# Ten of sixteen FFN weight slabs are loaded and split in the first FFN block instead of six of them in attention and four there

## What is computed

```python
# 1. attention: 4 batches, 8 heads, 576 positions, head size 64
out_d = sm_attn(q_d, k_d, v_d)              # on means of 4 positions
out_up = np.repeat(out_d, 4, axis=2)
mask = np.abs(pos[:, None] - pos[None, :]) < 4
out_local = np.matmul(softmax(where(mask, scale * q @ k.T, -1e9)), v)
x = out_up + out_local                      # 2304 tokens x 512
# 2. FFN: w_in 512 x 2048, w_out 2048 x 512
h = x @ w_in
g = h * np.tanh(log1p(exp(h)))
x = g @ w_out
# 3. each token goes through the best of 8 experts (512 x 1024, 1024 x 512)
```

## Time and profile before

| | us |
|---|---|
| median of 3 runs (946.82 to 948.1) | 946.95 |
| span of the profiled execution | 947.0 |
| TensorE busy | 871.4 (92%) |
| DVE busy | 510.1 (54%) |
| ACT busy | 429.1 (45%) |
| POOL busy | 231.5 (24%) |
| attention, to the first ffn_in | 0 to 214.5 |
| first FFN block, to the first ffn_out of the second | 214.5 to 291.5 |

### The profile page before, as it was taken

One profiled execution on the slowest core, in us unless ns is written; L12 is line 12 of the kernel. 1 busy time (PEld: TensorE's weight loads), 2 busy tenths in 40 slices (PEclk: granted clock), 3 DMA queues, 4 the chain that ended last, 5 costly groups with the idle time before them and its releaser, 6 DMA issues.

```text
span 947.0 us, 16050 instructions
## 1 busy us (share of the span) xinstructions
PE 871.4 (92%) x4845; PEld 734.7 (78%) x4846; DVE 510.1 (54%) x1023; ACT 429.1 (45%) x1186; POOL 231.5 (24%) x218
## 2 busy tenths in 40 slices
PE   4888888879999999999999999987799999999995
PEld 3666666668988988989989989975577777777773
DVE  6999999945756555555555555675741111111110
ACT  3777777754555445454454454452152222222121
POOL 2667666542230010010010001252311111111110
PEclk9899999969999999999999999998899999999997
DMA  5555555211100000000000000310331011110110
GB/s 117 149 147 149 148 148 147 56 43 45 45 1 34 1 1 33 0 0 33 0 0 33 0 0 34 115 64 34 127 107 45 22 44 44 43 39 28 44 44 12
DMA packets 88197, 51.57 MB, mean 54 GB/s; under 512 B 64480, under 2 KB 77280, under 8 KB 88160
## 3 DMA queue, kind: packets, MB, share of 16 engines
q1 hardware_dynamic: 85040, 41.16, 15.5%
q0 software_dynamic: 3120, 9.96, 3.1%
HBM read 41.67 MB, written 9.70 MB: 54 GB/s over the span
## 4 chain that ended last, share of the span: by engine, by line
PE 67%; DVE 14%; issue 6%; DMA 5%; ACT 3%; POOL 2%; DVEq 1%; SPq 0%; ACTq 0%; POOLq 0%
PE ps L1326 7%; PE ps L1327 7%; PE ps L1328 7%; PE ps L1302 6%; PE ps L1301 6%; PE ps L1307 6%; PE ps L1436 6%; PE ps L1438 6%; PE ps L1437 6%; DMA xg<-y_rows,gidx 4%; DVE smax L889 3%; DVE ssum L899 3%; DVE kdz L874 2%; DMA vwin<-in_v_dram 2%; PE ps L1227 1%
## 5 line engine op out<-in xcount | busy, mean ns | idle before, releaser
L988 DVE TENSOR_SCALAR Tb<-Eb 128x384 f32<-128x384 f32 x96 | 41.4, 431 | 133.9 <-ACT Eb L733 133.9
L733 ACT ACTIVATE Eb<-ps 128x384 f32<-128x384 f32 x96 | 47.1, 491 | 141.7 <-PE ps L1307 141.6
L1302 PE MATMUL ps<-xh,WA 128*128 128x384 f32 x288 | 98.3, 341 | 0.0
L663 ACT ACTIVATE prob<-ps,nmax 96x111 f32<-96x111 f32 (+1 forms) x256 | 87.8, 356 | 23.0 <-DVE nmax L893 22.7
L1301 PE MATMUL ps<-xh,WA 128*128 128x384 f32 x288 | 97.8, 340 | 0.0
L562 POOL TENSOR_TENSOR xl<-xT,xh 128x384 fp32r<-128x384 f32 x24 | 26.8, 1144 | 280.4 <-ACT xh L705 280.4
L1326 PE MATMUL ps<-WA,gh 128*128 128x512 f32 x216 | 87.1, 403 | 2.4 <-DVE gl L947 2.4
L1328 PE MATMUL ps<-WA,gl 128*128 128x512 f32 x216 | 85.4, 395 | 0.0
L1327 PE MATMUL ps<-WA,gh 128*128 128x512 f32 x216 | 85.2, 394 | 0.0
L1167 DVE TENSOR_TENSOR hTl<-ps,hTh 128x1024 fp32r<-128x1024 f32 x19 | 23.3, 1225 | 112.5 <-ACT hTh L796 112.5
L742 ACT ACTIVATE Rb<-Tb 128x384 f32<-128x384 f32 x96 | 50.5, 526 | 73.6 <-DVE Tb L990 73.6
(11 more groups left out here) (218 smaller groups left out, 2078.6 us busy)
## 6 DMA issues: line engine op xcount, KB each, us to landing
wsraw<-in_moe_w_dram SPq DMA_DIRECT2D x32, 256.0 KB, 3.2
vwin<-in_v_dram SPq DMA_DIRECT2D x32, 166.5 KB
qraw<-in_q_dram SPq DMA_DIRECT2D x32, 144.0 KB, 3.0
kraw<-in_k_dram SPq DMA_DIRECT2D x32, 144.0 KB, 3.1
vdraw<-in_v_dram SPq DMA_DIRECT2D x32, 144.0 KB
y_rows<-yrow SPq DMA_DIRECT2D x6, 768.0 KB, 3.6
wraw<-in_moe_w_in_dram SPq DMA_DIRECT2D x12, 256.0 KB, 5.6
wraw<-in_moe_w_out_dram SPq DMA_DIRECT2D x12, 256.0 KB, 3.5
```

Source lines behind the costliest of these rows:

```text
L663: last = act.activation(prob[0:np_, a.s6, n * w:(n + 1) * w], ps[0:np_, o:o + w], ACT.Exp, scale=sc, bias=nmax[0:np_, a.s6, n:n + 1], accu ...
L1302: pe.matmul(dst, lo, xh[:, kk, :], start=False, stop=False)
```

## The change

Only slabs 0 to 5 (NPRE = 6) are still loaded in attention, one in every second pair, into a wraw of half the size. Slabs 6 to 15 are loaded behind attention, and ACT casts one at the end of each of the first ten steps of the first FFN block. yrow and yT become one tensor, ystage, which is two stage buffers for slabs before it is used as yrow and yT; so two late slabs can be in flight. ACT gets a wait for w_lo ahead of the first xh, since xh lies where attention's buffers were. Where the parts of a slab lie (WA, WB) and what TensorE does stays.

```diff
-        wraw = alloc(att, "wraw", [P, 2, 2 * DM])
+        wraw = alloc(att, "wraw", [P, 2 * DM])
...
-        yrow = alloc(early, "yrow", [P, NS, DM])
-        yT = alloc(early, "yT", [P, NK, P])
+        ystage = alloc(early, "ystage", [P, NS * DM + NK * P])
+        yrow = ystage[:, 0:NS * DM].rearrange("p (s n) -> p s n", s=NS)
+        yT = ystage[:, NS * DM:NS * DM + NK * P].rearrange("p (a b) -> p a b", a=NK)
+        def slab_stage(j):
+            return ystage[:, (j % 2) * 2 * DM:(j % 2 + 1) * 2 * DM]
...
-        SLAB_LAG = 2
+        NPRE = NPAIR // 2 - 2
         def has_slab(m):
-            return not isinstance(m, int) or SLAB_LAG <= 2 * m < NWA + SLAB_LAG
+            return not isinstance(m, int) or 1 <= m <= NPRE
...
-                j, par = hp * B + (n - V_LAG), (n - V_LAG) % 2
-                split = hp * B + (n - V_LAG - 1)
                 load_v(hp, n - V_LAG)
-                if not static or j < NWA:
-                    wait(sp, w_lo, split)
-                    load_slab(j, wraw[:, par], wraw_in[par])
+                if (n - V_LAG) % 2 == 0:
+                    j = hp * (B // 2) + (n - V_LAG) // 2
+                    if not static or j < NPRE:
+                        wait(sp, w_lo, j)
+                        load_slab(j, wraw, wraw_in)
...
-            for j in range(NWA, NF):
-                sp.wait_ge(w_lo, j)
-                load_slab(j, yrow[:, 0:2, :].rearrange("p a b -> p (a b)"), wraw_in[j % 2])
+            for j in range(NPRE, NF):
+                wait(sp, w_lo, max(NPRE, j - 1))
+                load_slab(j, slab_stage(j), late_in[j % 2])
...
-                if has_slab(m) and dn % 3 == 1:
-                    split_lo(m * 2 + (dn // 3 - SLAB_LAG), wraw[:, dn // 3], True)
+                if has_slab(m) and dn == 1:
+                    split_lo(m - 1, wraw, True)
...
                 act.wait_ge(pooled, ROUNDS * NPAIR)
+                act.wait_ge(w_lo, NPRE)
                 x_part_hi(0)
...
-                    if first_block and j % 3 == 2 and NWA + j // 3 < NF:
-                        late_slab_hi(NWA + j // 3)
+                    if first_block and NPRE + j < NF:
+                        late_slab_hi(NPRE + j)
```

More of the change, by code:

```diff
@@ L133, in build @@
         Rb = alloc(early, "Rb", [P, 2, TB])
-        yrow = alloc(early, "yrow", [P, NS, DM])
-        yT = alloc(early, "yT", [P, NK, P])
+        ystage = alloc(early, "ystage", [P, NS * DM + NK * P])
+        yrow = ystage[:, 0:NS * DM].rearrange("p (s n) -> p s n", s=NS)
+        yT = ystage[:, NS * DM:NS * DM + NK * P].rearrange("p (a b) -> p a b", a=NK)
+        assert NS * DM + NK * P == 2 * (2 * DM)
+        def slab_stage(j):
+            return ystage[:, (j % 2) * 2 * DM:(j % 2 + 1) * 2 * DM]
         early.close()
@@ L273, in build @@
         v_due = sem("v_due")
-        wraw_in = [sem("wraw_in0"), sem("wraw_in1")]
+        wraw_in = sem("wraw_in")
+        late_in = [sem("late_in0"), sem("late_in1")]
         w_hi = sem("w_hi")
@@ L565, in _ @@
             x_part_lo(0)
-            for j in range(NWA, NF):
-                split_lo(j, yrow[:, 0:2, :].rearrange("p a b -> p (a b)"))
+            for j in range(NPRE, NF):
+                split_lo(j, slab_stage(j))
             with pool.Fori(1, NTB) as i:
@@ L746, in ffn_block @@
                         y_evac(i - 1)
-                    if first_block and j % 3 == 2 and NWA + j // 3 < NF:
-                        late_slab_hi(NWA + j // 3)
+                    if first_block and NPRE + j < NF:
+                        late_slab_hi(NPRE + j)
             def late_slab_hi(j):
-                split_hi(j, yrow[:, 0:2, :].rearrange("p a b -> p (a b)"), wraw_in[j % 2], 32 * (j // 2) + 32)
+                split_hi(j, slab_stage(j), late_in[j % 2], 32 * ((j - NPRE) // 2) + 32)
             def g_part_hi(c, par):
@@ L929, in step @@
                     copy_turned(dve.tensor_copy, dve, a, DVE_ROUND)
-                if has_slab(m) and dn % 3 == 0:
-                    j, par = m * 2 + (dn // 3 - SLAB_LAG), dn // 3
-                    dve.wait_ge(wraw_in[par], m * 32)
+                if has_slab(m) and dn == 0:
+                    dve.wait_ge(wraw_in, m * 32)
                     for which in range(2):
-                        last = dve.tensor_copy(w_part(j, which, 0, True), wraw[:, par, which * DM:(which + 1) * DM])
+                        last = dve.tensor_copy(w_part(m - 1, which, 0, True), wraw[:, which * DM:(which + 1) * DM])
                     last.then_inc(w_hi, 1)
```

## The result

The changed kernel takes 960.62 us (median of 4 runs, 957.95 to 963.65), the kernel before 946.88 (946.5 to 948.1). The ratio is 1.0149, with a 95% interval of 1.0123 to 1.0175: 13.7 us slower. The forecast was 960.3, in a range of 954 to 963. The profiled execution after spans 960.0 us against 947.0.

A forecast was written before the change was run, and what follows sets the result against it. Attention was taken as bound by the value-load loop over SP, loads and POOL, the FFN blocks by TensorE. 947.0 - 0.9 (attention) + 14.2 (first FFN block) = 960.3 us, range 954 to 963.

The forecast's parts named there:

- The sum, 960.3 us: Whole kernel: 947.0 us before, less 0.9 in attention, plus 14.2 in the first FFN block; own case 958.5 to 962.5, chance 0.70.
- Attention, -0.9 us: Attention: six slabs fewer to load and split gain 0.9 us, the middle between bounds of 0 and 1.7.
- the loop of the loads: Attention: vdraw and vwin loads issued by SP, their landing and POOL's additions form one loop of 11.92 us a pair.
- Rival 1: Attention: DVE sets the pace, so each of six pairs gains 1.2 us, 7.2 in all, giving 954.0 us; chance 0.14.
- Rival 2: Attention: SP's queue sets the pace; some 3.3 us of slab issue leaves each of six pairs, giving 941.3 us; chance 0.03.
- One sign: Attention, profile after: POOL's sums (L524's successor) were to be 11.6 to 12.0 us apart in all pairs.
- The first slab, +4.3 us: First FFN block's start: ACT waits 1.7 us for the first late slab, so ffn_out(0) starts 4.3 us late, at 227.7.
- Nine steps of 5.30 us: First FFN block, ffn_out(0) to ffn_out(9): steps of 5.30 us against TensorE's 4.19; ffn_out(9) at 275.4 instead of 261.15.
- Rival 3: First FFN block: the slab work is hidden in each step, only the start loses 2.8 us, giving 948.9 us; chance 0.04.
- The clock, 0 to 1.6 us: First FFN block: TensorE's clock may fall during its first wait, costing 1.6 us at most; 0 was taken.
- Rival 4: First FFN block: the clock stays at 1.2 GHz beyond the first gap, +4 us a step, +42 over ten; chance 0.06.

## Why the prediction was right, point by point

**The sum, 960.3 us.** It missed the median by 0.3 us. The four runs spread over 5.7 us, so a hit as close as that is luck; that the loss is 12 to 17 us is not. The prediction took span and time as one, but in the runs on record the time is 1.7 to 2.0 us above the span. It did no harm, as 947.0 was the median of the times too.

**Attention, -0.9 us.** 1.1 us measured at the first ffn_in, and 0.2 us as the mean of three kernels with the same attention. The bounds of 0 and 1.7 held it; that the middle came so near is luck. The upper bound put the 0.29 us by which the last three pairs are shorter down to the slabs. They are 11.45 us apart after the change and the twelve before them 11.88, so the lead is not smaller with half the slabs gone: it isn't theirs, and zero was the right bound. That the loop of the loads sets the pace in the kernel before and the changed one is shown from three sides: opening it in either of two places shortens a pair (to 10.06 and 10.97 us), slowing its load lengthens the pair by 6.0 us, by as much as SP's issue of the load (9.31 instead of 3.35) and by as much as the load by the estimate, and taking slabs from DVE does nothing that shows. Rival 1 falls. Rival 2, a slab's issue on SP as the price, falls with the same rows: the pairs without a slab aren't 2.4 us shorter, POOL idles longer in them. One sign was set too narrow: the sums on POOL were to be 11.6 to 12.0 us apart in all pairs. They are 11.36 to 12.83 apart, and were 11.39 to 12.42 before.

**The first slab, +4.3 us.** ACT waited 1.48 us (forecast 1.7); ffn_out(0) started 4.75 us behind the cast (4.80), at 226.90, 13.51 us after the first ffn_in, before 8.90: 4.6 us. Moving the casts one step later took 3.6 of them back.

**Nine steps of 5.30 us.** ffn_out(9) came at 274.57. The forecast had 275.4 less the 0.9 of attention, 274.5. Against the first ffn_in it is 14.5 us late, forecast 14.2; the 0.3 us are the first slab's. The reading of the last block, where the same pattern stood already, gave this number to 0.1 us a step. The step as the sum of cast, POOL's pair and the way back (1.20 + 2.66 + 1.43) comes from the runs; the prediction had only the sum of 5.30. Rival 3, the slab hidden, needs POOL quiet: 4.19 us apart with the small subtraction.

**The clock, 0 to 1.6 us.** It fell to 0.50 behind the first gap, for some 3 us, and matmuls of 128x512 took 0.63 us instead of 0.39. The steps of ffn_out(0) to (2) took it up: the gap before ffn_out(2) is 0.36 us, half a microsecond less than in the steps after it. So 0 was the right value. Rival 4 fell: at gaps of 0.85 us the clock is 1.00 through 30 us.

**What the prediction passed over.** It read the 55 GB/s of vwin and used it only to say that slabs don't slow it. That the rate itself is low, and what it is worth, 28 us, was there in the same row.

## What to carry to other kernels

Before work is taken from an engine that looks full, follow one turn of the loop that feeds it, over all queues and the load's landing: an engine may be busy in the profile because its instructions wait, and then work taken from it becomes idle time elsewhere. Work moved under a full TensorE costs by the chain of one step, not by the busy time of an engine: three pieces in a row that exceed TensorE's step are paid in every step, and it is paid back nowhere. Look at the partition count of each load on such a chain: 111 in one piece or in 96 and 15 made 28 us here, while cutting it in 74 and 37 cost 97.

## What was not expected of the hardware

The issue of a transfer on SP's queue takes longer behind slow ones: the first half of a slab's load took 2.95 us to issue behind vwin loads of 111 partitions, 2.86 behind 74 and 37, and 0.40 behind 96 and 15. And the busy time of DVE in attention hardly fell when half of its slab casts went (with the loop open 85.31 of 90 us with twelve slabs, 83.83 with six), as some small operations got longer in their place (nmax of 96x6 took 295 ns from 40 to 140 us, then 438, on average; ssum of 96x6 got shorter, 563 and 491): such a share says little of the work in it. Why the ten runs of the kernel with two vdraw buffers scatter over 13 us, when 13 of the kernel before on the same chip scatter over 6, stays open; the mean granted clock goes with the time, 0.972 and 0.974 in the two fastest and 0.961 in the slowest, which doesn't say which of them is the cause.
